# Up-projections by Strassen's seven products, one layer after the other, x in DRAM between them

## The reference, cut to what matters

```
qn, kn = q / norm(q, axis=1), k / norm(k, axis=1)        # q, k, v: 1 x 6016 x 256
a = softmax(kn.T @ qn / tau)                             # 256 x 256
x = v @ a                                                # 6016 x 256
h = x @ w_in1;  x = (h * sigmoid(1.702 * h)) @ w_out1    # w_in: 256 x 2048, w_out: 2048 x 256
h = x @ w_in2;  y = where(h > 0, h, exp(min(h, 0)) - 1) @ w_out2
```

## Time and profile before

| | us |
|---|---|
| median of three runs | 1127.82 (1124.95 to 1132.54) |
| the profiled execution | 1128.4 |
| its span, first to last instruction | 1126.7 |
| PE busy | 1109.5, 98% |
| DVE busy | 802.6, 71% |
| ACT busy | 433.5, 38% |
| POOL busy | 39.3, 3% |

### The profile page before, as it was taken

One profiled execution on the slowest core, in us unless ns is written; L12 is line 12 of the kernel. 1 busy time (PEld: TensorE's weight loads), 2 busy tenths in 40 slices (PEclk: granted clock), 3 DMA queues, 4 the chain that ended last, 5 costly groups with the idle time before them and its releaser, 6 DMA issues.

```text
span 1126.7 us, 14340 instructions
## 1 busy us (share of the span) xinstructions
PE 1109.5 (98%) x4902; PEld 910.9 (81%) x4902; DVE 802.6 (71%) x1271; ACT 433.5 (38%) x688; POOL 39.3 (3%) x23
## 2 busy tenths in 40 slices
PE   9899999999999999999999999999999999999997
PEld 8677788888888888888888888888888888889887
DVE  8879967667766776676766666776776677667765
ACT  7553225325324424424423423522532442442443
POOL 0063200000000000000000000000000000000000
PEclk9999999999999999999999999999999999999999
DMA  9653000020020010001002002002002001001001
GB/s 322 229 150 94 1 1 1 1 37 0 0 37 0 0 33 4 0 11 26 0 0 37 0 0 37 0 0 37 0 0 37 0 0 33 1 1 20 1 1 33
DMA packets 108967, 33.33 MB, mean 30 GB/s; under 512 B 98704, under 2 KB 102800, under 8 KB 108944
## 3 DMA queue, kind: packets, MB, share of 16 engines
q1 hardware_dynamic: 108944, 33.04, 12.1%
HBM read 26.87 MB, written 6.16 MB: 29 GB/s over the span
## 4 chain that ended last, share of the span: by engine, by line
PE 92%; DVE 5%; SPq 1%; issue 0%; DMA 0%; ACT 0%; DVEq 0%; ACTq 0%
PE bank L637 30%; PE bank L639 30%; PE bank L638 30%; DVE g_hi L585 2%; PE bank L652 1%; DVE g_lo L587 1%; DVE gated L578 1%; DVE sumsq L472 1%; DMA qk<-in_k_dram 0%; PE bank L707 0%; PE bank L702 0%; PE bank L703 0%; SPq L228 0%; PE bank L645 0%; DVE rq_row L534 0%
## 5 line engine op out<-in xcount | busy, mean ns | idle before, releaser
L578 DVE SCALAR_TENSOR_TENSOR gated<-act_out,bank 128x512 f32<-128x512 f32 (+1 forms) x384 | 258.8, 674 | 247.9 <-ACT act_out L413 141.7
L637 PE MATMUL bank<-g_hi,wo_hi 128*128 128x512 f32 (+1 forms) x768 | 300.5, 391 | 4.8 <-DVE g_lo L587 4.8
L638 PE MATMUL bank<-g_lo,wo_hi 128*128 128x512 f32 (+1 forms) x768 | 298.5, 389 | 0.0
L639 PE MATMUL bank<-g_hi,wo_lo 128*128 128x512 f32 (+1 forms) x768 | 298.3, 388 | 0.0
L587 DVE TENSOR_TENSOR g_lo<-gated,g_hi 128x512 fp32r<-128x512 f32 (+1 forms) x384 | 268.2, 698 | 13.2
L408 ACT ACTIVATE act_out<-bank 128x512 f32<-128x512 f32 (+1 forms) x192 | 113.3, 590 | 382.8 <-PE bank L639 361.3
L411 ACT ACTIVATE act_out<-bank 128x512 f32<-128x512 f32 (+1 forms) x192 | 113.2, 590 | 273.3 <-PE bank L639 273.3
L585 DVE CAST g_hi<-gated 128x512 fp32r<-128x512 f32 (+1 forms) x384 | 175.8, 458 | 39.6 <-PE bank L639 0.5
L637 PEld LDWEIGHTS bank<-g_hi,wo_hi 128*128 128x128 f32 x768 | 144.1, 188 | 37.7 <-DVE g_lo L587 5.5
L639 PEld LDWEIGHTS bank<-g_hi,wo_lo 128*128 128x128 f32 x768 | 144.4, 188 | 31.6
L638 PEld LDWEIGHTS bank<-g_lo,wo_hi 128*128 128x128 f32 x768 | 144.4, 188 | 30.6
(11 more groups left out here) (94 smaller groups left out, 628.3 us busy)
## 6 DMA issues: line engine op xcount, KB each, us to landing
qk<-in_q_dram SPq DMA_DIRECT2D x15, 384.0 KB, 4.0
qk<-in_k_dram SPq DMA_DIRECT2D x15, 384.0 KB, 5.1
out_dram<-y_blk SPq DMA_DIRECT2D x44, 128.0 KB, 2.5
v_blk<-in_v_dram SPq DMA_DIRECT2D x40, 128.0 KB, 3.1
stage<-in_moe_w_in_dram SPq DMA_DIRECT2D x8, 512.0 KB, 5.8
stage<-in_moe_w_out_dram SPq DMA_DIRECT2D x8, 512.0 KB, 3.9
y_blk<-in_v_dram SPq DMA_DIRECT2D x4, 128.0 KB, 4.1
v_blk<-in_v_dram SPq DMA_DIRECT2D x4, 96.0 KB, 2.9
```

What stands on the lines that cost most here:

```text
L578: nc.vector.scalar_tensor_tensor(out=f, in0=act_out[:, m % 2, 0:w], scalar=1.0, in1=h_ps[m % HBANKS][:, 0:w], op0=ops[0], op1=ops[1]).then ...
L637: nc.tensor.matmul(out_ps, w_hi, x_hi, start=start, stop=False)
L638: nc.tensor.matmul(out_ps, w_hi, x_lo, start=False, stop=False)
L639: return nc.tensor.matmul(out_ps, w_lo, x_hi, start=False, stop=stop)
```

## The change

The attention and the a_w product remain. What follows them is ordered anew.

**Pairs and units.** Tokens are now cut into NP = 6 pairs of tiles (2 x 512, the last 2 x 448). A unit U is a pair with two chunks of features; a segment s is a pair in one layer, UNITS = 8 units. Segments 0 to 5 are layer one of all pairs, 6 to 11 layer two, 96 units in all.

**Seven products.** The up-projection of a unit is a product of 2 x 2 blocks: four weight blocks with four blocks of activations (two halves of the inputs, two tiles). It is computed in Strassen's form as Winograd wrote it, with seven block products, each three matmuls. The weights' blocks are A11, A12, A22 and the sums S1 to S4, the activations' blocks X11, X21, X22 and the differences T1 to T4; each is split in `hi` and `lo`. The down-projection is as before, 6 matmuls per tile and chunk, 24 a unit. The four results of a unit are called H11, H22, H21 and H12.

**How the sums form.** Products 1, 6, 7 and 4 accumulate in one bank (`chain`), and ScalarE copies it to SBUF after products 1, 6 and 7 (u1, u2, u3). H11 = u1 + product 2; H22 = u3 + product 5; H12 = u2 + (products 5 and 3); H21 is the bank at the end. VectorE adds; H11 and H12 are written back to PSUM in place. `chain` has two banks that alternate, the other two sums one bank each.

**x between the layers.** ScalarE takes the accumulators out of PSUM into `xo`, SP stores them to `x_scratch` in DRAM and loads them later as `raw`, 1 MB per pair.

**Weights.** One place in SBUF holds the layer's weights; those of layer two replace them quarter by quarter in segments 5 and 6. The S-sums are made by POOL (the first by VectorE), the splits of `w_up` by ACT and DVE, of `w_out` by ACT and POOL.

The loops over units are written out flat on all engines. The diff, cut to the new functions that order the work:

```diff
+        blk = [sb(ctx, f"blk_{x}", [P, S_RING, T], F32R) for x in ("hi", "lo")]      # S_RING = 10
+        chain = banks[0:2]
+        sum11, sum2212 = banks[2], banks[3]
+        acc = [banks[4:6], banks[6:8]]
...
         @block.sync
+            def next_v(p, tile):
+                sp.wait_ge(c_vt, 2 * p + tile)
+                load_v(blocks, p, tile, c_v)
+            def store_x(p):
+                for tile in range(2):
+                    sp.wait_ge(c_evac, 4 * p + 2 * tile + 2)
+                    w = width(p)
+                    sp.dma_start(x_dram[p][:, :, tile, 0:w], xo[:, :, tile, 0:w]).then_inc(c_xst, 16)
+            def load_x(p):
+                sp.wait_ge(c_blo, N_BLOCKS * (NP + p))
+                sp.wait_ge(c_xst, 32 * (p + 1))
+                w = width(p)
+                sp.dma_start(raw[:, :, :, 0:w], x_dram[p][:, :, :, 0:w]).then_inc(c_x, 16)
+            def store_y(p):
+                for tile in range(2):
+                    sp.wait_ge(c_y, KC * (2 * p + tile + 1))
+                    for b in range(P // B):
+                        sp.dma_start(rows_of(out, row_of(p, tile), width(p), b),
+                                     part_of(blocks, width(p), b)).then_inc(c_yst, 16)
...
+            for s in range(1, NP - 1):
+                store_x(s - 1)
+                next_v(s + 1, 0)
+                next_v(s + 1, 1)
+            store_x(NP - 2)
+            load_x(0)
+            for fb in range(FB):
+                sp.wait_ge(c_uplo, 3 * (FB + fb))
...
+            store_x(NP - 1)
+            load_x(1)
+            for p in range(NP - 2):
+                store_y(p)
+                load_x(p + 2)
...
         @block.scalar
+            def evacuate(s, tile):
...
+                for d in range(KC):
+                    nc.scalar.mul(xo[:, d, tile, 0:w], acc[tile][d][:, 0:w],
+                                  0.5 if s < NP else 1.0).then_inc(c_evac, 1)
+            def side(U):
+                if u == 0:
+                    block_hi(s, T4)
+                    block_hi(s, X22)
+                if s < SEGS - 1:
+                    if u == 4:
+                        block_hi(s + 1, X11)
+                        block_hi(s + 1, X21)
+                    if u == 5:
+                        block_hi(s + 1, T2)
+                    if u == 7:
+                        block_hi(s + 1, T1)
+                        block_hi(s + 1, T3)
+            def unit(U):
+                if U:
+                    g_hi(U - 1, H21)
+                if 0 < U < ALL:
+                    copy_u1(U)
+                if u == 1 and s >= 1:
+                    evacuate(s - 1, 1)
+                if U:
+                    nonlinear(U - 1, H12)
+                if U < ALL:
+                    nonlinear(U, H11)
+                if U and U - 1 < LAYER:
+                    g_hi(U - 1, H12)
...
+                    copy_u2(U)
+                if U < LAYER:
+                    g_hi(U, H11)
+                side(U)
+                if U:
+                    copy_u3(U)
+                weights(U)
+                nonlinear(U, H22)
+                if u == 0 and s >= 1:
+                    evacuate(s - 1, 0)
+                nonlinear(U, H21)
+                g_hi(U, H22)
...
         @block.vector
+            def y_of(p, tile):
+                dve.wait_ge(c_evac, 4 * (NP + p) + 2 * tile + 2)
+                if 2 * p + tile:
+                    dve.wait_ge(c_yst, V_LOAD * (2 * p + tile))
+                transpose_y(p, tile, [xo[:, d, tile, 0:width(p)] for d in range(KC)], blocks)
+            def side(U):
+                if u == 0:
+                    block_lo(s, T4)
+                    block_lo(s, X22)
+                if s > NP:
+                    if u == 1:
+                        y_of(s - 1 - NP, 0)
+                    if u == 3:
+                        y_of(s - 1 - NP, 1)
+                if s < SEGS - 1:
+                    if s + 1 < NP and u in (1, 2):
+                        transpose_v(s + 1, u - 1, blocks, c_v, V_LOAD * (2 * s + 2 + u - 1))
+                    if u == 3:
+                        t_of(s + 1, T1)
+                        t_of(s + 1, T2)
+                    if u == 4:
+                        block_lo(s + 1, X11)
+                        block_lo(s + 1, X21)
+                    if u == 5:
+                        t_of(s + 1, T3)
+                        block_lo(s + 1, T2)
+                    if u == 6:
+                        t_of(s + 1, T4)
+                    if u == 7:
+                        block_lo(s + 1, T1)
+                        block_lo(s + 1, T3)
+            def unit(U):
+                if U:
+                    sum12_of(U - 1)
+                    g_lo(U - 1, H22)
+                if U < ALL:
+                    sum11_of(U)
+                if U:
+                    g_lo(U - 1, H21)
+                    gate(U - 1, H12)
+                if U < ALL:
+                    gate(U, H11)
+                if U:
+                    if U - 1 >= LAYER:
+                        g_hi(U - 1, H12)
+                    g_lo(U - 1, H12)
...
+                if U >= LAYER:
+                    g_hi(U, H11)
+                g_lo(U, H11)
+                side(U)
+                sum22_of(U)
+                weights(U)
+                gate(U, H22)
+                gate(U, H21)
...
         @block.tensor
+            def unit(U):
+                product1(U)              # waits for the gate of H21 two units back
+                product2(U)              # gate of H11 of the unit before
+                down_both(U - 1, H11)    # its g_lo
+                product6(U)              # u1
+                down_both(U - 1, H22)
+                product5(U)              # gate of H12 of the unit before
+                product7(U)              # u2
+                down_both(U - 1, H21)
+                down(U - 1, H12, 0)
+                product4(U)              # u3
+                down(U - 1, H12, 1)
+                product3(U)              # the sum for H22
```

More of the change, by code:

```diff
@@ L30 @@
 BANK = 512
-HBANKS = 4
-LAG = 3
 GELU_ALPHA = 1.702
[L36 to L42, removed]
+A11, A12, A22, S1, S2, S3, S4 = range(7)
+X11, X21, T2, T1, T3, T4, X22 = range(7)
+N_BLOCKS = 7
+H11, H22, H21, H12 = range(4)
+F_OF = {H11: 0, H22: 1, H21: 1, H12: 0}
+TILE_OF = {H11: 0, H22: 1, H21: 0, H12: 1}
 def attention_and_two_mlps(nc, q, k, v, tau, w_in1, w_out1, w_in2, w_out2, out):
@@ L159, in attention_and_two_mlps @@
         c_gate = sem("c_gate")
-        c_ghi = sem("c_ghi")
+        c_ghi = [sem(f"c_ghi{x}") for x in ("11", "22", "21", "12")]
         c_glo = sem("c_glo")
[L162 to L167, removed]
-        c_y = sem("c_y")
[L172 to L190, removed]
+        c_d = sem("c_d")
+        c_evac = sem("c_evac")
+        c_xst = sem("c_xst")
+        c_y = sem("c_y")
+        c_yst = sem("c_yst")
         V_LOAD = 16 * (P // B)
@@ new lines, in _ @@
+            load_v(blocks, 0, 1, c_v)
+            for qu in range(2):
+                load_w_out(qu, w_out1, qu)
+            def next_v(p, tile):
[6 more added lines that the diff above has]
+                    sp.dma_start(x_dram[p][:, :, tile, 0:w], xo[:, :, tile, 0:w]).then_inc(c_xst, 16)
@@ L313, in _ @@
+            dn_lo(0)
+            for n in range(1, FB):
+                s_of(n)
+                dn_lo(n)
+            for n in range(FB, 2 * FB):
+                s_of(n)
+                dn_lo(n)
         @block.scalar
@@ L446, in _ @@
-            assert EVAC_AT not in between
-            run(seg1, {EVAC_AT: lambda: split_x_direct(seg1, xT, acc_b, T)} | between)
-            def run_pair(a, b):
-                run(a, {EVAC_AT: lambda: evacuate_x(a), SPLIT_AT: lambda: split_v_hi(b.tile, vT, b.width)})
-                run(b, {EVAC_AT: lambda: split_x_hi(b)})
-            with nc.Fori(0, LOOP, engines=[act.engine], hint_back_edge=True) as t:
-                run_pair(*pair(t))
-            run_pair(end[0], end[1])
-            run(end[2], {EVAC_AT: lambda: split_x_direct(end[2], vT, acc_a, TL)})
@@ L460, in _ @@
+            for U in range(ALL + 1):
+                unit(U)
         @block.vector
         def _(dve):
-            dve.sem_inc(c_y, 1)
             nc.vector.memset(scores[:, :, :], 0.0).then_inc(c_zero, 1)
@@ L625, in _ @@
[L625 to L630 removed]
+            transpose_v(0, 1, blocks, c_v, V_LOAD)
+            block_lo(0, X11)
+            t_of(0, T1)
@@ L783 @@
+            for n in range(4):
+                a_w(n)
+            product1(0)
+            product2(0)
+            a_w(4)
+            product6(0)
+            product5(0)
+            a_w(5)
+            product7(0)
+            a_w(6)
+            a_w(7)
+            product4(0)
+            product3(0)
+            for U in range(1, ALL):
+                unit(U)
+            for x in (H11, H22, H21, H12):
+                down_both(ALL - 1, x)
 _INS = ['q', 'k', 'v', 'tau', 'moe_w_in', 'moe_w_out', 'moe2_w_in', 'moe2_w_out']
```

782 lines of the change are left out of this document (481 added, 301 removed).

## The result

The changed kernel takes 1165.75 us (median of four runs, 1164.8 to 1167.87) against 1128.94 before (four runs): 1.033 times as long, interval 1.029 to 1.037. The forecast was 1180, 1.046 times. The profiled execution has a span of 1166.0 us.

What follows compares the result with a forecast made beforehand. TensorE (10.43 us a unit) bounds layer one; in layer two, a ring of VectorE and ScalarE with side work in series. Terms 78 + 82 + 338 + 85 + 95 + 408 + 79 + 13 give 1178, plus 1.7 around the span: 1180 us, range 1100 to 1225.

Steps and rivals of the forecast that it cites:

- The ring: Layer two, each unit: VectorE and ScalarE wait for each other in turn; 10.21 us against TensorE's 10.43, side work added.
- The sums on PSUM: VectorE sums with one PSUM source and PSUM output: 0.69 us, 0.61 to the next operation (bounds 0.61 and 0.75).
- my third rival: Whole kernel costlier: no overlap of VectorE operations, 1196 us, up to 1240 with dearer sums or late fetch; chance 0.10.
- The wait for x: Unit 3 of segments 7 to 10: VectorE waits for the load queued behind stores of y; 9 us in each segment.
- The estimate of 4.4 us: The 1 MB load of x by the skill's formula, about 2.0 us plus bytes over 436 GB/s; sum 6 us less.
- TensorE's pace: Each full unit: 45 matmuls at 0.2317 us take 10.43 us, so a segment of 8 units takes 83.4 us.
- v in layer one: Segments 1 to 4: next pair's v loads only behind the store of x; 1 us charged per segment (bounds 0 and 3).
- The weights: Preparing layer-two weights on POOL and VectorE: +9 us in segment 0, +12 in segment 5, 4.5 in segment 6.
- The start: From eT at 55.1 us to unit 1 at 78 (bounds 74 and 84); H22 sum and product 3 end at 77.6.
- product 4 waits for T4's split (75.0): First unit: product 4 is held until VectorE's split of T4 at 75.0 us; H22 sum and product 3 end at 77.6.
- The sum: Whole kernel: start, segments and end add to 1178 us of span, 1180 us with 1.7 us around it.
- the first (TensorE bound throughout, 1062): Whole kernel: TensorE stays the bound in both layers, 1062 us (1062 to 1095); chance 0.13.

Runs made afterwards that it cites:

- The experiment: Changed kernel with the next pair's x load issued between the stores of y's first and second tile: 1132.5 us, ratio 1.0053.
- the best version: Changed kernel with early x and v loads, side work behind the H22 sum, first T4 and X22 splits ahead, first tile's evacuation behind copy three: 1085.1 us, ratio 0.9617.

## Why the prediction was right, and where its sizes were off

**The ring, right.** Built from distances of starts in the earlier trace rows, it was 10.21 us and is 10.06; the three idle places are there; side work is in series (11.43 by my account, 11.30 measured). Three experiments hold it from three sides: added work on VectorE costs its full length in layer two and almost nothing in layer one, work moved into the idle place costs almost nothing, and a shorter ScalarE step frees the layer.

**The sums on PSUM, right.** H11 and H12 sums take 0.70 and 0.69 us, with 0.60 to 0.61 to the next, the lower end of my bounds. The Trainium skill (VectorE: DVE Perf Modes, "The DRAIN you can't avoid") says that the next operation does not start until the pipe is empty, and adds that one that is not "held" starts earlier. In the unit shown above the full operations that follow each other directly start 0.60 to 0.66 us apart at 0.68 to 0.70 long. So the trace, as in the earlier trace rows, agrees with the addition; my third rival took the first half alone.

**The wait for x, right.** 9 us predicted, 8.2 to 8.4 measured, four times. The 1 MB load lands in 5.5 us in the median, where I took 6 from rows. The estimate of 4.4 us by the Trainium skill (DMA: Bandwidth & Descriptors, its two cost components) was too low here; the page gives that sum as a fit for DMAs issued through GpSimd, and this load is issued by SyncE. The experiment gives 33 us for 33.1 us of waits, so in layer two none of them had been absorbed.

**TensorE's pace, 2% too slow.** A unit takes 10.20 us, not 10.43: 0.2267 us per matmul against the 0.2317 of the earlier trace rows. Over the 39 units of 512 columns in layer one that is 9 us. Why the matmuls come closer together was not tested.

**v in layer one, too small.** My 1 us a segment was what I thought would be left of the wait after the slack of layer one; without the wait the segments are 9.9 us shorter in all (the early load of v), so 2.5 each were left. The wait itself was in the account: v at about 9 us into the unit, wanted by the transpose at 6.3. In segment 1, unit 1 begins (its H12 sum) at 176.58; v comes 9.5 us later and was wanted 5.8 us later:

```profile
175.48 3.88 SPq L315 DMA_DIRECT2D x_scratch<-xo  x2
179.41 3.95 SPq L282 DMA_DIRECT2D blocks<-in_v_dram  x4
186.10 1.25 DVE L721 STREAM_TRANSPOSE raw<-blocks 128x1024 f32<-128x1024 f32 x1 [3.72 <-DMA blocks<-in_v_dram]
```

The four loads took 3.95 us to issue where the earlier trace rows has 2.95. What was mis-sized was the slack.

**The weights, too large.** I put 9, 12 and 4.5 us on segments 0, 5 and 6. Segment 5 took 81.2 us against 85. In segment 0 the H22 sums of units 0 and 8 lie 86.0 apart, where 7 x 10.43 + 9 and the first unit gave about 91. POOL itself was busier than in my account: its work for the second quarter takes 7.55 us (four rows, 98.56 to 106.30) against 4.9. I had added each hold of VectorE by POOL in full, though layer one has slack for some; that this is the reason was not tested.

**The start, the largest miss.** 76.3 us predicted for the first H22 sum, 87.1 measured. The step that failed is "product 4 waits for T4's split (75.0)": I followed VectorE's queue and left out ScalarE's, where the first tanh stands behind two a_w evacuations and a 1.03 us cast. VectorE waits 6.97 us for it, and gate, `g_lo` and T4 come behind: T4's split runs at 84.9. Some 1.6 us of this wait are the lower clock shown above, which I did not have in the account either.

**The sum.** In us, measured less predicted: start +10.8, segment 0 -5, segments 1 to 5 -5.6, segment 6 -4.4, segments 7 to 10 -7.6, last segment and end about 0; together -12, the 1166.0 of span against 1178. The total is nearer than its terms, and part of that is luck: the start was 10.8 too short while the rest was 22.6 too long, and inside segments 1 to 4 the pace (7 too much) hid that v cost 6 more than I had. Of the rivals, the first (TensorE bound throughout, 1062) is not what this kernel does, but 1085 is reached once the waits and the order are mended, so the saved matmuls are real: 288 at 0.23 us are 66 us, and the best version has 44 of them.

## What to carry to other kernels

When two in-order engines hand work to each other several times in an iteration, write out one iteration by starts, not by busy time: its length can exceed any engine's work (here 11.3 us, with VectorE idle for 2.2), and everything that stands in series in it costs its full length, as long as no third engine is slower than the ring. Side work belongs behind the instruction that another engine is waiting for. A load queued behind a store waits for whatever the store waits for; put it where its own conditions are met.

## What was not expected of the hardware

- Matmuls of 512 columns follow each other every 0.2267 us in layer one of the changed kernel and 0.2317 before, both at a granted clock of 1.00. The cause was not looked for.
- POOL's operation on 512 columns took 1.72 us in the mean (27.2 us for 16), more than half of the 2.42 that 1024 columns took before, which fits POOL being held in its turn when VectorE works on SBUF. It was not tested:

```profile
L386 POOL TENSOR_TENSOR w_dn_lo<-stage,w_dn_hi 128x512 fp32r<-128x512 f32 x16 | 27.2, 1723 | 100.5 <-ACT w_dn_hi L496 100.5
```
- The granted clock was 0.95 in segments 7 to 10, where TensorE waited up to 9.6 us in each for the H22 sum, and 1.00 with these waits gone; the prediction expected 1.00 throughout. The time of the lowered clock itself did not show: 12.7 us of unit 2 and 8.3 of wait make 21.0, and 21.1 was measured.
